# Banded attention on one Trainium2 core: the order of turning, copying and inverting inside a two-tile step

## What is computed

```python
scores = scale * np.matmul(q, k.transpose(0, 1, 3, 2))
keep = is_global | is_local            # the first 8 positions, and the last 96
bias = -slopes[:, None, None] * dist[None, :, :]
scores = np.where(keep, scores + bias[None], -1000000000.0)
scores = scores - np.max(scores, axis=-1, keepdims=True)
a = np.exp(scores)
a = a / (np.sum(a, axis=-1, keepdims=True) + 1e-09)
x = np.matmul(a, v)                    # then _moe_ref(x), then _moe2_ref(x)
```

## Time and profile before

| | |
|---|---|
| median of 3 runs | 1050.72 us (1049.54 to 1051.94) |
| the profiled execution | 1050.72 us, of it the span of the records 1049.0 us |
| PE busy in the span | 919.3 us (88%) |
| DVE busy | 680.0 us (65%) |
| ACT busy | 451.2 us (43%) |
| POOL busy | 191.1 us (18%) |
| TensorE clock granted, mean | 0.919 of full |
| DMA | 129.40 MB, mean 123 GB/s |

### The profile page before, as it was taken

The page is one execution under the profiler, slowest core; times in us unless marked ns, Lnnn a source line. Parts: engine busy times, 40 slices in busy tenths (PEclk is TensorE's granted clock), DMA queues, the critical chain, the costliest instruction groups (busy, mean ns, idle before and its releaser), DMA issues.

```text
span 1049.0 us, 22340 instructions
## 1 busy us (share of the span) xinstructions
PE 919.3 (88%) x6394; PEld 773.8 (74%) x6397; DVE 680.0 (65%) x1823; ACT 451.2 (43%) x982; POOL 191.1 (18%) x247
## 2 busy tenths in 40 slices
PE   6889999884999999999999985444599999999994
PEld 4767777773788888888888873333398989899993
DVE  4778888758766968869877784555554645463521
ACT  3778888746344352535525350000042524343410
POOL 1222322300111111111111110000203212321211
PEclk8899999987899999999999996555699999999998
DMA  9577677342351524515334251000135353635100
GB/s 213 110 160 169 161 172 165 85 178 81 111 201 41 209 69 171 200 50 200 121 129 150 93 190 57 2 2 2 34 108 209 123 198 133 220 115 203 42 31 31
DMA packets 146567, 129.40 MB, mean 123 GB/s; under 512 B 102464, under 2 KB 114752, under 8 KB 146368
## 3 DMA queue, kind: packets, MB, share of 16 engines
q1 hardware_dynamic: 137696, 99.68, 31.8%
q0 software_dynamic: 8800, 28.84, 8.1%
HBM read 107.79 MB, written 20.71 MB: 122 GB/s over the span
## 4 chain that ended last, share of the span: by engine, by line
PE 72%; DVE 9%; issue 6%; SPq 5%; DMA 3%; DVEq 2%; ACT 1%; POOL 0%; ACTq 0%; POOLq 0%
PE ps_o L1298 14%; PE ps_s L1275 14%; PE ps_o L1640 9%; PE ps_s L1624 6%; PE ps_pT L1624 6%; PE ps_s L1640 4%; PE ps_t L1801 3%; DMA qn<-in_q 2%; PE ps_pT L1286 2%; PE ps_o L509 2%; SPq L2053 2%; SPq L2072 1%; PE ps_t L461 1%; PE ps_t L1261 1%; PE ps_s L478 1%
## 5 line engine op out<-in xcount | busy, mean ns | idle before, releaser
L1298 PE MATMUL ps_o<-w_split_parts,hs 128*128 x696 | 169.2, 399 | 6.3 <-issue 6.3
L1275 PE MATMUL ps_s<-w_split_parts,xs 128*128 x696 | 165.8, 394 | 1.1 <-ACT xs L1367 1.1
L1298 PEld LDWEIGHTS ps_o<-w_split_parts,hs 128*128 128x128 f32 x696 | 130.1, 190 | 33.9 <-issue 7.1
L1485 DVE SCALAR_TENSOR_TENSOR product<-y_sb,wg_all 128x512 bf16<-128x512 f32 x224 | 145.8, 689 | 11.4 <-issue 6.7
L1275 PEld LDWEIGHTS ps_s<-w_split_parts,xs 128*128 128x128 f32 x696 | 128.9, 189 | 26.6 <-issue 1.3
L820 ACT ACTIVATE arena_p<-arena_p,min_s 128x256 f32<-128x256 f32 (+1 forms) x192 | 92.3, 484 | 29.6 <-DVE min_s L688 28.8
L1640 PE MATMUL ps_o<-w_split_parts,hs 128*128 128x512 f32 x384 | 94.1, 397 | 0.0
L1476 DVE TENSOR_TENSOR w_split_parts<-raw,w_split_parts 128x1024 f32 (+1 forms) x68 | 78.7, 1221 | 20.3 <-ACT w_split_parts L1386 19.0
L1640 PEld LDWEIGHTS ps_o<-w_split_parts,hs 128*128 128x128 f32 x384 | 70.2, 188 | 15.9 <-ACT hs L1674 2.9
L1720 DVE TENSOR_TENSOR w_split_parts<-raw,w_split_parts 128x1024 fp32r<-128x1024 f32 x56 | 68.6, 1225 | 18.7 <-ACT w_split_parts L1682 18.5
L1375 ACT ACTIVATE hs<-ps_pT 128x512 fp32r<-128x512 f32 x58 | 31.7, 597 | 113.1 <-PE ps_pT L1286 113.1
(11 more groups left out here) (307 smaller groups left out, 1690.5 us busy)
## 6 DMA issues: line engine op xcount, KB each, us to landing
raw<-in_moe_w SPq DMA_DIRECT2D x32, 2048.0 KB, 9.2
y_rows<-y_sb POOLq DMA_DIRECT2D x31, 256.0 KB, 2.3
kn<-in_k SPq DMA_DIRECT2D x32, 192.0 KB, 3.5
qn<-in_q SPq DMA_DIRECT2D x32, 192.0 KB, 3.6
vn<-in_v SPq DMA_DIRECT2D x32, 192.0 KB, 2.9
x_rows<-arena_x SPq DMA_DIRECT2D x96, 64.0 KB, 1.6
va<-in_v SPq DMA_DIRECT2D x32, 120.0 KB, 2.7
wg_rows<-in_moe_w_gate SPq DMA_DIRECT2D x1, 2048.0 KB, 7.6
```

The costliest lines, as they stand in the source:

```text
L1275: last = nc.tensor.matmul(ps_s[:, f, :], xs[:, a, c * P:(c + 1) * P], weights(par, w, cols), start=(n == 0), stop=(n == len(passes) - 1))
L1298: last = nc.tensor.matmul(ps_o[:, 0, :], hs[:, a, c * P:(c + 1) * P], weights(par, 2 + w, slice(c * DM, (c + 1) * DM)), start=(n == 0), st ...
L1485: nc.vector.scalar_tensor_tensor(product[:, e % 2, :], y_sb[:], 1.0, wg_all[:, e, :], ALU.mult, ALU.mult, accum_out=log_now[:, e:e + 1])
```

## The change

In `two_pairs` of the three engines: (a) on PE `turn` stands behind `turn_probs` instead of ahead of `turn_back`; the groups are no longer split in front and rest. (b) On ACT `high_qk` stands behind the second pair of exponentials, where it stood behind the first. (c) The copies out of `ps_pT`: ACT makes those of tiles 3, 7, 9 and 11, DVE the other eight, where each made six; on ACT the copy keeps its place between the two pairs of exponentials. (d) `invert` runs once a step on 4 columns and stands at the start of DVE's step, ahead of the first `bias_scores`, where it ran once a pair on 12 columns behind it.

```diff
+        KEPT_BY_ACT = (3, 7, 9, 11)
...
-        def each_turn(it, t, first, last_one, which):
...
-        FRONT, MORE = slice(0, 1), slice(1, None)
...
# pe_banded
                         score(it, t + 1)
-                    for pair, nth, par, g in each_turn(it, t, first, last_one, FRONT):
-                        turn(pair, nth, par, g)
                     if t >= 2:
                         turn_back(it, t - 2)
                     elif not first:
                         turn_back(it - 1, t - 2 + TWOS)
                     turn_probs(it, t)
+                    for nth, g in turns_of(first, last_one).get(t, ()):
+                        turn(it * 2 + nth + 1, it + (nth + 1) // 2, (nth + 1) % 2, g)
                     if t >= 1:
                         value(it, t - 1)
                     elif not first:
                         value(it - 1, TWOS - 1)
-                    for pair, nth, par, g in each_turn(it, t, first, last_one, MORE):
-                        turn(pair, nth, par, g)
...
# dve_banded
-            def invert(it, par):
-                s = sums_b[:, 12 * par:12 * par + 12]
-                dve.wait_ge(exped, it * 24 + 12 * par + 12 + ATT0)
+            def invert(it, t):
+                s = sums_b[:, 4 * t:4 * t + 4]
+                dve.wait_ge(exped, it * 24 + 4 * t + 4 + ATT0)
...
-                    more = t + 1 < TWOS or not last_one
-                    if more:
+                    before_it, back = (it, t - 2) if t >= 2 else (it - 1, t - 2 + TWOS)
+                    done_one = t >= 2 or not first
+                    if done_one:
+                        invert(before_it, back)
+                    if t + 1 < TWOS or not last_one:
                         bias_scores(it, 2 * t + 2)
-                    if t % 3 == 2:
-                        invert(it, t // 3)
...
-                    keep_turned(it, 2 * t)
-                    for pair, _, par, g in each_turn(it, t, first, last_one, slice(None)):
-                        low_qk(pair, par, g)
+                    for s in (2 * t, 2 * t + 1):
+                        if s not in KEPT_BY_ACT:
+                            keep_turned(it, s)
+                    for nth, g in turns_of(first, last_one).get(t, ()):
+                        low_qk(it * 2 + nth + 1, (nth + 1) % 2, g)
...
# act_banded
                         exp(it, 2 * t + 2)
-                    for pair, _, par, g in each_turn(it, t, first, last_one, FRONT):
-                        high_qk(pair, par, g)
-                    keep_turned(it, 2 * t + 1)
-                    if more:
+                    for s in (2 * t, 2 * t + 1):
+                        if s in KEPT_BY_ACT:
+                            keep_turned(it, s)
+                    if t + 1 < TWOS or not last_one:
                         exp(it, 2 * t + 3)
+                    for nth, g in turns_of(first, last_one).get(t, ()):
+                        high_qk(it * 2 + nth + 1, (nth + 1) % 2, g)
                     if t >= 1:
                         copy_cols(it, t - 1)
```

More of the change, by code:

```diff
@@ L436, in turns_of @@
             return {0: [(0, 0), (0, 1), (0, 2)] if first else [(0, 2)], 1: [(1, 0)], 2: [(1, 1)], 3: [(1, 2)], 4: [(2, 0)], 5: [(2, 1)]}
-        def each_turn(it, t, first, last_one, which):
-            return [(it * 2 + nth + 1, it + (nth + 1) // 2, (nth + 1) % 2, g)
-                    for nth, g in turns_of(first, last_one).get(t, [])[which]]
-        FRONT, MORE = slice(0, 1), slice(1, None)
         def width(i):
@@ L720, in two_pairs @@
                 for t in range(TWOS):
-                    more = t + 1 < TWOS or not last_one
-                    if more:
-                        bias_scores(it, 2 * t + 2)
-                    if t % 3 == 2:
-                        invert(it, t // 3)
[L726 to L729, removed]
-                    if more:
-                        bias_scores(it, 2 * t + 3)
-                    keep_turned(it, 2 * t)
-                    for pair, _, par, g in each_turn(it, t, first, last_one, slice(None)):
-                        low_qk(pair, par, g)
+                    before_it, back = (it, t - 2) if t >= 2 else (it - 1, t - 2 + TWOS)
[3 more added lines that the diff above has]
+                    if t + 1 < TWOS or not last_one:
+                        bias_scores(it, 2 * t + 2)
+                    if done_one:
+                        norm(before_it, back)
+                    if t + 1 < TWOS or not last_one:
+                        bias_scores(it, 2 * t + 3)
+                    for s in (2 * t, 2 * t + 1):
[3 more added lines that the diff above has]
+                        low_qk(it * 2 + nth + 1, (nth + 1) % 2, g)
                 if last_one:
                     for t in (TWOS - 2, TWOS - 1):
+                        invert(it, t)
                         norm(it, t)
@@ L851, in two_pairs @@
                         copy_cols(it - 1, TWOS - 1)
-                    for pair, _, par, g in each_turn(it, t, first, last_one, MORE):
-                        high_qk(pair, par, g)
                 if last_one:
```

## The result

The changed kernel is slower: 1101.52 us, median of four runs (1100.81 to 1103.03), beside 1051.33 (1049.54 to 1052.86) for the one before on the same chip, a ratio of 1.048 with the 95% interval 1.0459 to 1.0501. The forecast was 1095, with a range of 1076 to 1112. The profiled execution took 1102.12 us, where that of before took 1050.72: 51.4 more. The last `norm` of the attention starts at 262.84 where it started at 212.61, so 50.2 of it lies in the attention, and 1.2 behind it, where nothing was changed.

A forecast was written before the change was run, and what follows sets the result against it. PE sets the pace before; afterwards a ring through DVE and ACT bounds each step. The 36 steps give +40.0, five others +5.5, the start -1.5: +44.0 on 1050.7, so 1095, range 1076 to 1112.

The forecast's parts named there:

- The ring: Attention step: first bias, ACT's exponentials and copy, high part, low part, `invert`, next bias in sequence; 5.0 us a step.
- Steps 0 to 5: The six attention steps of a steady turn, each summed from its pieces; together 30.0 us against 23.3.
- `invert`, the term that was mis-sized: Inversion with two drains at the head of DVE's step: 0.65 us in each step.
- The upper bound: 41 steps with 0.3 us more for the "issue" gap and ACT waits: 1107; with some clock loss, 1112.
- Width: DVE's inversion on 4 columns: nearly all cost fixed, 0.65 us as for 12; by width alone 0.22.
- Outside the 36 steps: The other twelve attention steps: +5.5 for five with a group, -1.5 at the start, 0 for the last five.
- The first two steps: Start of the attention: about 3 us of data waits, half hidden by `turn` behind the probabilities, -1.5 us.
- the main cost: ACT's `high_qk` behind the second exponentials puts 0.98 to 1.5 us of exponentials and copy into the ring.
- (a) gives little: PE's `turn` behind `turn_probs` gets 0.9 to 1.0 us of cover, but PE no longer bounds, except in the start.
- Only load: Attention: only engine load counts, DVE's work 3.78 us a step, below 3.89; time stays 1050.7; 7 in 100.
- PE freed: Attention: `turn` waits go, PE stays the bound at 3.69 us a step; -9 us, 1042; 5 in 100.
- The clock: Attention: idle PE's clock drops to 0.5, 2.4 us on top in 23 steps; 1150; 8 in 100.

The follow-up runs named there:

- `invert` in the wait: From the changed kernel, the six inversions a turn moved ahead of the low part, where DVE waits for the high part: 1074.13 us, ratio 1.0196.
- after: The changed kernel with all four parts of the change, against the kernel before: 1101.52 us, ratio 1.048.
- `turn` early: From the changed kernel, only PE's `turn` put back ahead of turning back and of the probabilities, high part still late: 1110.28 us, ratio 1.0553 of the kernel before.

## Why the prediction was right, point by point

- **The ring.** Shown. It took the place of PE as the bound, with the waits that were named: DVE for the high part, no wait for scores, ACT for the bias. Opening it at the high part gives back 37 us.
- **The lengths of the steps.** Steps 0 to 5 were to be 4.61, 5.48, 4.58, 5.05, 5.48, 4.83. The timeline gives 4.75, 5.64, 4.64, 5.22, 5.65, 5.01: the order is right, and all are long by 0.06 to 0.18, 0.9 a turn. Over 36 steps that makes +45.15 for +40.0.
- **`invert`, the term that was mis-sized.** It was taken as 0.65. In the loop it measures 155.64 to 156.45, 0.81, and 165.50 to 166.31, 0.81: six times 0.16 is 0.96, the whole of the 0.9, and the other terms together came 0.1 short of their sum. The row it came from has `norm` behind the inversion, 0.41 from start to start; here the first bias stands there, and it takes 0.58 (155.87 to 156.45). It is the bias behind a drain that is late: straight behind a low part, in the run with `invert` in the wait, a bias followed after 0.23, without a gap. The upper bound held "the 'issue' gap of 0.16 us that stands between a low part and the next instruction": right in size, but not the cause: in three runs a bias starts behind a low part without that gap. The 0.1 to 0.15 that the same bound adds on ACT stands in no row, and ACT's pieces came as they were read (0.62, 1.00, 0.47 for the copy, 0.99).
- **Width.** That 4 columns cost what 12 do is shown: the inversion took 0.18 for 0.23, the add 0.16 for 0.17. By the Trainium skill, "VectorE: DVE Perf Modes", section "Rules for kernel authors", each chained instruction pays its flush whatever its neighbour. The trace agrees in that the count of instructions sets the price and not the width; it does not in that the neighbour makes no difference, since the pair with its drains takes 0.61 us ahead of `norm` and 0.81 ahead of a bias.
- **Outside the 36 steps** +4.0 was forecast, and the attention shows 50.2 less 45.15, +5.1. The first two steps gave a gain, but of 0.7 us for the 1.5 forecast: the first bias of the third step starts at 33.87, before at 34.57.
- **What each part costs.** Here the text was only half right. (b) is the main cost: alone it is +44, 4.5 of it the clock, and taking it out of after gives 37. But the parts do not add. "(a) gives little" was wrong by itself: alone it costs 10.6, because the high part, where it stood, then waits for the transposes; with (b) it gives 20 back, because `turn` no longer holds up the probabilities and the falls of the clock go with that. (d) was priced too low on the closed ring, by the 0.16 of above (27.2 us between its two places over the 36 steps), and costs 6.4 without it, 3.3 of which is the stall next to POOL. (c) gives 0.9 a turn, forecast 1.
- **The rivals.** Only load: out, since the same load with another place of the high part or of `invert` differs by 37 and 29 us. (Its sum counts 30 more inversions; 48 for 16 are 32, which changes nothing in it.) PE freed: out, the low part starts 3.16 to 3.99 us into DVE's step, and the rival needed less than 2.9; PE waits more. The clock: it fell in five of the turns, but did not set the time. After's windows of 2 us at two such falls, columns as above:

```profile
138.00:140.00 2.00, 0.83 (x10) 0.63 (x7) 0.60 (x1) 1.52 (x6) 2.00 (x2) 0.85 0.40 118
140.00:142.00 2.00, 2.00 (x12) 2.00 (x11) 1.52 (x10) 0.46 (x3) 0.95 (x1) 0.50 0.48 119
...
144.00:146.00 2.00, 2.00 (x24) 1.83 (x22) 1.01 (x4) 0.69 (x3) 0.00 (x0) 1.00 0.41 68
...
170.00:172.00 2.00, 1.52 (x7) 1.53 (x8) 1.22 (x5) 0.42 (x2) 1.85 (x2) 0.53 0.34 98
```

In 138 to 140 PE was busy 0.83 us and the clock fell; in 140 to 142 it was 0.50, 1.2 GHz, with PE full; by 144 it was back. The same comes five times from 40 to 240 us, at the end of step 4 and the start of step 5. Steps 1 and 4 are made of the same pieces, and step 4 alone has a fall in it (170 to 172): it took 5.65 (166.31 to 171.96), step 1 without one 5.64. Step 5 takes 5.01 with the fall and, from 202.84, without. PE has a quarter of each step to spare, and the ring does not notice. So "at clock 1.00" was wrong, and the 8 in 100 for a clock that costs stood for something that did not come in this kernel. It is no empty rival: where `turn` stands ahead of the probabilities and is held up for the bank, a fall lengthens its step by 0.2 to 1.1 us, 4.5 us in all with the high part late alone and 3.2 with `turn` early. That is far from the 55 us that it was priced at. The Trainium skill, "TensorE: Matmul & The Clock Gate", section "A second HAM failure mode: psum-queue depth-cycling", tells of short pauses that let the clock swing. The trace shows such swings; in after they cost nothing to be seen, and in the two other runs what the steps above show.

## What to carry to other kernels

Before an instruction is moved, follow its result round through all engines back to its own queue: if it comes back to itself, the step cannot be shorter than the sum, however idle the engines are. A small fixed cost, here 0.8 us for two short instructions and their drains, is nearly free outside such a ring or in a wait, and costs its full length times the steps on it. Parts of a change that touch the same ring do not add: each has to be tried with the others and without. And when waits are compared between two runs, the view must be the same: `turn` waits 8.6 us for data by its matmuls alone and 12.7 with its weight loads.

## What was not expected of the hardware

- The two drained 4-column instructions of `invert` took 0.81 us from start to the first bias in the loop, 0.61 to `norm` in the loop, and 0.67 to the first bias in the code of the first turn, which stands written out (37.56 to 38.23 in after). Only 0.34 of it is counted as busy. What makes the difference was not tried.
- In the loop the clock fell to 0.50 after 2 us with PE busy 0.83 (138 to 140), and stayed at 1.00 in other stretches with PE as idle: 0.84 of 2 us from 153 to 155. What decides between them these runs do not show.
- An add on 128x4 values, 0.16 us otherwise, took up to 3.49 us on DVE while POOL filled and numbered tiles of 1024 columns; its whole length counts as busy, so no wait shows it.
